# Moving the cast of the weights' high parts from VectorE to ScalarE in a fused attention and MLP kernel, with three small moves beside it

## The reference, cut to what matters

```python
# attention: batch 4, heads 8, sequence 576, head dim 64
scores = scale * q @ k^T ; log_f = log(clip(f)) ; cum = cumsum(log_f)
scores = where(causal, -1e9, scores + cum[:, None] - cum[None, :])
attn = softmax(scores) ; x = attn @ v            # (2304 tokens, 512)
# MLP: d_model 512, d_ff 2048
h = x @ w_in ; g = h * sigmoid(1.702 * h) ; x2 = g @ w_out
# soft mixture of experts: 32 slots, 8 experts, 1024 wide
logits = x2 @ phi
slots  = softmax(logits, over tokens)^T @ x2
slots  = relu(slots @ w1[e]) @ w2[e]             # 4 slots for each expert
out    = softmax(logits, over slots) @ slots
```

## Time and profile before

| What | us |
|---|---|
| median of three runs | 772.56 (771.88 to 776.73) |
| the profiled execution's own time | 776.32 |
| its span, from first to last instruction | 774.5 |
| TensorE busy | 718.1 (93%) |
| VectorE busy | 495.7 (64%) |
| GpSimd busy | 411.4 (53%) |
| ScalarE busy | 370.8 (48%) |

### The profile page before, as it was taken

The page is one execution under the profiler, slowest core; times in us unless marked ns, Lnnn a source line. Parts: engine busy times, 40 slices in busy tenths (PEclk is TensorE's granted clock), DMA queues, the critical chain, the costliest instruction groups (busy, mean ns, idle before and its releaser), DMA issues.

```text
span 774.5 us, 15770 instructions
## 1 busy us (share of the span) xinstructions
PE 718.1 (93%) x6024; PEld 680.7 (88%) x6024; DVE 495.7 (64%) x1383; ACT 370.8 (48%) x903; POOL 411.4 (53%) x439
## 2 busy tenths in 40 slices
PE   3999979999999898999999989999999999998993
PEld 3888878999899898999999989999999999995562
DVE  5799857778877756786767667867553454424323
ACT  4777855464646464555556564646342133111113
POOL 4355356474757755565658554857385576530000
PEclk9899989999999999999999999999999999998998
DMA  4333322333333332233332423332213445498986
GB/s 102 105 91 105 94 63 80 94 82 91 94 93 94 93 81 74 84 98 90 94 99 52 119 54 93 94 93 79 64 48 114 158 133 194 140 396 300 385 332 244
DMA packets 96506, 96.65 MB, mean 125 GB/s; under 512 B 61296, under 2 KB 61296, under 8 KB 96432
## 3 DMA queue, kind: packets, MB, share of 16 engines
q1 hardware_dynamic: 96432, 95.66, 40.2%
HBM read 90.84 MB, written 4.79 MB: 123 GB/s over the span
## 4 chain that ended last, share of the span: by engine, by line
PE 69%; DVE 14%; ACT 5%; issue 3%; DMA 3%; POOL 2%; SPq 1%; DVEq 0%; POOLq 0%
PE mb L1204 47%; PE yb L1057 5%; PE zb L1076 5%; PE xb L1103 4%; DVE ptl L838 2%; DMA ring_b<-in_moe_w 2%; DVE prob L832 2%; ACT prob L684 2%; DVE kl L800 2%; DVE qs L796 2%; PE xb L1037 1%; POOL xl L633 1%; PE mb L1255 1%; DVE hid L921 1%; PE yb L1059 1%
## 5 line engine op out<-in xcount | busy, mean ns | idle before, releaser
L1204 PE MATMUL mb<-xh,wih 128*128 128x288 f32 x512 | 159.2, 311 | 11.0 <-DVE hid L921 5.2
L1204 PE MATMUL mb<-gh,woh 128*128 128x288 f32 x512 | 157.2, 307 | 4.2 <-DVE x2t L928 4.2
L1204 PE MATMUL mb<-xh,wil 128*128 128x288 f32 x512 | 151.9, 297 | 0.0
L1204 PE MATMUL mb<-xl,wih 128*128 128x288 f32 x512 | 151.9, 297 | 0.0
L1204 PE MATMUL mb<-gl,woh 128*128 128x288 f32 x512 | 151.0, 295 | 0.0
L1204 PE MATMUL mb<-gh,wol 128*128 128x288 f32 x512 | 150.9, 295 | 0.0
L643 POOL TENSOR_TENSOR gl<-hid,gh 128x288 fp32r<-128x288 f32 x128 | 114.4, 899 | 58.3 <-ACT gh L723 57.4
L684 ACT ACTIVATE prob<-prob,m_row 64x576 f32<-64x576 f32 (+4 forms) x160 | 96.4, 604 | 62.4 <-DVE m_row L818 61.9
L660 POOL TENSOR_TENSOR wol<-stage,woh 128x512 fp32r<-128x512 f32 x64 | 82.7, 1292 | 72.1 <-DVE woh L790 72.1
L660 POOL TENSOR_TENSOR wil<-stage,wih 128x512 fp32r<-128x512 f32 x64 | 83.1, 1300 | 71.4 <-DVE wih L790 71.4
L921 DVE SCALAR_TENSOR_TENSOR hid<-gate,mb 128x288 f32<-128x288 f32 x128 | 57.7, 451 | 98.8 <-ACT gate L729 97.3
(11 more groups left out here) (196 smaller groups left out, 1424.7 us busy)
## 6 DMA issues: line engine op xcount, KB each, us to landing
stage<-in_moe_w_in SPq DMA_DIRECT2D x64, 256.0 KB, 3.0
stage<-in_moe_w_out SPq DMA_DIRECT2D x64, 256.0 KB, 2.6
ring_a<-in_moe_w SPq DMA_DIRECT2D x16, 1024.0 KB, 7.3
ring_b<-in_moe_w SPq DMA_DIRECT2D x14, 1024.0 KB, 12.5
cum_b<-cum_dram SPq DMA_DIRECT2D x32, 288.0 KB, 3.7
qk_in<-in_q SPq DMA_DIRECT2D x32, 144.0 KB, 3.0
qk_in<-in_k SPq DMA_DIRECT2D x32, 144.0 KB, 3.4
v_in<-in_v SPq DMA_DIRECT2D x32, 128.0 KB, 3.2
```

Source lines behind the costliest of these rows:

```text
L1204: ins = mm(bank[:, 0:HALF], a[:, t, P * (j % 4):P * (j % 4) + P], x[:, t, cols], start=(i == 0), stop=(i == 11))
```

## The change

- The cast of the weights' high part moves from VectorE's list to ScalarE's: in the first batch at the head of slots 3 to 6, later behind ScalarE's part of units 0, 1, 3 and 4 (behind the tanh and the cast `gh` in kind 0; in kind 1 ScalarE has nothing before it but one `gh` at unit 0).
- `late`, VectorE's sum of a head's output halves, moves from behind `score(1)` and `pt(1)` to directly behind `pt(0)`.
- The low part of the last pair of heads (`xs[3]`, VectorE) is made behind one more unit in slot 8 of the batches that carry units.
- The constant products go from (7, 16) to (9, 3, 14): nine new ones ahead of the first wait of the end chain, three in place of seven, fourteen in place of sixteen.

```diff
-BUSY = (7, 16)
+BUSY = (9, 3, 14)
@@ batch_steps, the list of VectorE and POOL
-            steps += (f() + vsplit + pt(0) + f() + score(1) + pt(1) + late + f() + score(2) + pt(2)
+            steps += (f() + vsplit + pt(0) + (late if engine == "dve" else []) + f() + score(1) + pt(1) + f() + score(2) + pt(2)
                       + qk + f() + score(3) + pt(3) + dup + f() + norm + f() + early
-                      + (early_x + f() + pv + xs[3] if s == 0 else f()) + f(2))
+                      + (early_x + f() + pv + f() + xs[3] + f() if s == 0 else f(3)))
@@ ScalarE
+            def w_split(order, which, t):
+                hi = (wih, woh)[which]
+                act.wait_ge(w_dma[t % 2], 16 * ((order >> 1) + 1) if isinstance(order, int) else (order - t % 2) * 8 + 16)
+                nc.scalar.copy(hi[:, t, :], stage[:, t % 2, :]).then_inc(w_hi, 1)
...
+                elif st[0] == "split":
+                    w_split(st[1], 0, st[1])
...
+                    pieces = w_pieces(u, is_last(m))
+                    if pieces and j in SPLIT_AT:
+                        t = SPLIT_AT.index(j)
+                        w_split(m * 32 + 8 * pieces[0] + pieces[1] + t, pieces[1] // 4, t)
@@ VectorE
-            def w_split(order, which, t):
-                hi = (wih, woh)[which]
-                dve.wait_ge(w_dma[t % 2], 16 * ((order >> 1) + 1) if isinstance(order, int) else (order - t % 2) * 8 + 16)
-                nc.vector.tensor_copy(hi[:, t, :], stage[:, t % 2, :]).then_inc(w_hi, 1)
...
-                elif st[0] == "split":
-                    w_split(st[1], 0, st[1])
...
-                pieces = w_pieces(u, last)
-                if pieces and j in SPLIT_AT:
-                    t = SPLIT_AT.index(j)
-                    w_split(m * 32 + 8 * pieces[0] + pieces[1] + t, pieces[1] // 4, t)
@@ TensorE, after the last unit
             turn_logits(last_turn)
+            busy(BUSY[0])
             pe.wait_ge(t_dve, 1)
             pe.wait_ge(token_out, 1 + (BATCH - 1) * QT + 2)
             tr(zb[0:SLOTS, 0, 0:P], gmax[:, :], ident[:, :]).then_inc(t_pe, 1)
             turn_last(4)
-            busy(BUSY[0])
+            busy(BUSY[1])
             pe.wait_ge(t_dve, 3)
             mm(zb[:, 1, 0:SLOTS], ones[0:SLOTS, :], dmax[:, :], start=True, stop=True).then_inc(t_pe, 1)
-            busy(BUSY[1])
+            busy(BUSY[2])
```

## The result

The changed kernel takes 764.39 us (median of four runs, 762.25 to 766.44) against 772.62 us before (four runs). The medians differ by 8.2 us. The ratio is 0.9882, with a 95% interval of 0.9837 to 0.9927: 1.2% faster, which is 9.1 us. The profiled execution took 765.15 us with a span of 763.3 us; that of before took 776.32 us, one of its slower executions, so the two traces differ by 11.2 us where the medians differ by 8.2.

A forecast was written before the change was run, and what follows sets the result against it. TensorE was taken to bound the kernel, with only its waits, lower-clock stretches and end chain to shorten. 3.6 + 2.0 + 1.6 + 1.2 + 0.4 + 0.9 - 2.5 = 7.2 us, so 772.6 - 7.2 = 765.4 us; range 759 to 772.5, its own 761 to 769.

The forecast's parts named there:

- Where the gain can come from: TensorE: only its waits (some 13 us in all for x2t, hid, q/k transposes), lower-clock stretches and end chain can shorten.
- The low part of the last pair: Slot 8: one more unit before VectorE's subtraction lets the bank be read first; 3.6 us gained, bounds 2.0 and 3.6.
- The sum of the halves: Transposes of q and k: an earlier sum of output halves removes three TensorE waits; 2.0 us gained, bounds 0.5 and 2.5.
- The casts: Weight casts leaving VectorE shorten x2t waits by 1.6 us and hid waits by 1.2; on ScalarE they lose 2.5.
- the rival of the clock: End chain: added products keep the clock at 2.4 GHz, saving 3.8 us instead of 0.9; 762.5 us, chance 0.20.
- the nine waits whose chain runs through it: Seven hid and two x2tok waits of TensorE end last through ScalarE; casts there lengthen them, 2.5 us lost.
- The constant products: End chain: nine new products cost nothing in idle time, fewer later ones save 0.9 us together.
- The first batch: Four casts leave a nearly always busy VectorE in the first batch; 0.4 us gained, bounds 0 and 1.7.
- the third rival's: The case of the clock staying up in the end chain: 3.8 us saved there instead of 0.9, chance 0.20.
- ScalarE giving it back: Stalls move to ScalarE's queue, a late pth or tanh in each slot of batches 1 to 3; 771 us, chance 0.23.
- The slower rival: Kind 0 with attention: woh casts before tanh stall TensorE, 0.40 us at each of 48; 782 us, chance 0.08.
- a sooner dispatch not reaching the end: End: if weight DMAs were bandwidth-bound from the first load, a sooner dispatch brings nothing; little chance, no separate number.

The follow-up runs named there:

- the two runs with all lists changed: The changed kernel itself, 764.39 us, and the changed kernel with the old constant products (7, 16) at the old places, 763.67 us.

## Why the prediction was right, and which of its steps were not

The forecast was 765.4 us by a gain of 7.2; the time is 764.4 by a gain of 8.2. That the total came out so near is luck in good part: two terms were wrong by 3.6 us and 6 us, in opposite directions.

- **Where the gain can come from: right.** The windows said that TensorE's waits and its clock were all there was. Of the 8.0 us in the units, 5.6 + 5.2 + 2.5 - 3.4 - 3.2 = 6.7 are waits of the three kinds named, less 0.5 of new waits for `x2tok` (L1125), and the stretch at the lower clock near 125 is worth up to 1.7.
- **The low part of the last pair: wrong in size.** The term was 3.6 us and the part alone brought 0.0 (1.0004). The step that failed is "because a unit of cover lies behind it". What stands behind that unit in the kernel before is a cast of `w_in`; it lasts 1.43 us beside POOL's work and takes the place of the wait removed. Beside the casts the move does clear slot 8, which the casts alone leave at 1.35, 1.35 and 0.48 us, but waits of much the same sum stand at the start of the next batches. For this move and the sum of the halves together, the traces of the casts alone (590.5 us for the units) and of the two runs with all lists changed (589.8 and 588.0) leave 0.7 and 2.5 us.
- **The sum of the halves: right in size**, 2.0 forecast and 1.9 measured (0.6 to 3.2), with the waits at L1037 gone as described. That `hid` waits take over a part of them was not in the term.
- **The casts: the mechanism right, the balance wrong.** 3.2 - 2.5 = 0.7 us was forecast and 6.8 measured alone. By the trace of that run, the `x2t` waits gave 2.2 (1.6 forecast) and the `hid` waits 2.0 (1.2). The waits at L1037 gave 1.5, which was booked under the sum of the halves alone. The stretch near 125 gave up to 1.7, which was in no term; it was named only with the rival of the clock. And ScalarE gave back the 0.5 us of new `x2tok` waits that show, not 2.5: the nine waits whose chain runs through it did not each grow by part of a cast, and the seven for `hid` shrank. The run with 26 us more of copies in kind 0 is no slower either.
- **The constant products: right in size, not resolved.** 0.9 us forecast, 1.2 measured with an interval that reaches to nothing, and none against the old numbers in the changed kernel. The dispatch started 3.2 us after the first product of the end chain (692.12 and 695.29), where 4.5 was forecast; the difference is the clock, which the rival below had up.
- **The first batch:** 0.4 forecast, 0.5 in the traces.
- **The range of its own** does not follow: the bounds of the terms as given add up to a gain of 13.7 us at the one end (more with the third rival's) and a loss of 1.6 at the other, so 759 to 774, not 761 to 769.
- **The rivals.** ScalarE giving it back shows in one place, the start of a batch (1.77 us near 427; 0.62 and 1.11 in two other traces with these lists), not in each slot. The slower rival is refuted: its casts plus 0.41 us still fit. The clock did stay up through the dispatch, in all nine profiles with the new numbers and in one of five with the old ones, and shortened that stretch by 3.7 us where 3.8 was said. How much of it reached the end differs. In the four traces where the clock did not fall before 740 us either, 62.3 to 63.0 us follow the dispatch, as in before (62.5), and all of it did. Where it fell in the first expert's product, 63.1 to 65.7 follow. So what this rival says of the clock came true, and what it says of the time did not: the products alone bring at most 2.6 us, where it had 3.8. The chance that I gave to a sooner dispatch not reaching the end was small, and its mechanism, loads bound by bandwidth from the first on, is not what the traces show.

What stays open: how much the moved low part is worth beside the casts (the changed kernel without it was not run), whether the constant products bring anything, why the clock falls in the first expert's product in some executions and not in others, and whether the later splits of `w_in` help.

## What to carry to other kernels

When several waits of the bounding engine trace back to one engine's queue, price the removal of work from that queue first, and price a reordering within it by what stands next in the list. On VectorE's full queue the reordering shortened one wait from 1.49 to 0.33 us and gained nothing measurable; with the casts gone it cleared the slot, and waits came up in the next batch. Compare waits by place and not by their sum: two traces had 3.4 us of `x2t` waits each, and none of the large ones in common. Ask of each wait whether a stretch at the lower clock follows it, since that goes with the wait. And the busy time of an engine that waits for the bounding one is a poor guide to what an added instruction costs: ScalarE waited 79 us for TensorE here, and 26 us more of work cost nothing that the runs could tell.

## What the runs showed of the hardware

- VectorE's 128x512 cast out of memory lasted 0.41 to 1.47 us in the trace of before. The 31 of 128 that took over 0.6 us all began while a subtraction of POOL was running; of the 97 others 42 did. ScalarE's lasted 0.60 to 0.64 us, 48 of them begun beside POOL's.
- The same two instructions of VectorE (`xl`) and POOL (`gl`) overlapped in two orders. With VectorE's first by 0.04 us they took 0.76 and 1.38 us (changed kernel); with POOL's first by 0.24 us they took 1.37 and 1.00 (the last low part alone).
- Around a wait of TensorE of 4.3 us the granted clock was 0.50 for 3.4 to 6.8 us in twelve traces, and never in two with constant products in the wait. Behind a wait of 1.8 to 1.9 us near 124 it was 0.50 for 3.4 us in six traces, and with that wait at 1.4 to 1.6 us it stayed at 1.00 in eight.
- Constant products ahead of the first step of the end chain, with fewer behind: in none of nine traces did the clock fall before the dispatch was over, and in four of five without them it did. In five of the nine it fell in the first expert's product instead, and in four not before 740 us.
